# Routing of a two-stage mixture kernel: products of three token tiles taken together, gate steps of three chunks put behind the places

## What is computed

```python
# attention: B, H, S, D = 2, 8, 576, 64, causal softmax, plus a memory read, mixed by a gate
x = attn_out.transpose(0, 2, 1, 3).reshape(1152, 512)
h = x @ w_in                                   # 512 -> 2048
g = where(h >= 1, h, where(h <= -1, 0, (h + 1) ** 2 / 4))
x2 = g @ w_out                                 # 2048 -> 512
logits = x2 @ w_gate                           # 8 experts
expert_idx = argmax(logits, axis=1); gate_w = softmax(logits)[expert_idx]
for i in range(N):                             # a place in the expert's list, up to capacity 288
    e = expert_idx[i]
    if counts[e] < capacity: disp[e, counts[e]] = x2[i]; pos[i] = counts[e]; counts[e] += 1; keep[i] = True
y = relu(disp @ w1) @ w2
out[i] = gate_w[i] * y[expert_idx[i], pos[i]]  if keep[i] else 0
```

## Time and profile before

| | |
|---|---|
| median of 3 runs | 320.57 us (320.23 to 320.6) |
| profiled execution | 319.95 us, of it the traced span 318.2 us |
| TensorE matmul busy | 309.4 us (97% of the span), 2737 matmuls |
| VectorE busy | 212.0 us (67%) |
| ScalarE busy | 143.4 us (45%) |
| GpSimd busy | 122.3 us (38%) |
| granted TensorE clock | 1.00 (mean of the core), which is 2.4 GHz |

### The profile page before, as it was taken

One profiled execution on the slowest core, in us unless ns is written; L12 is line 12 of the kernel. 1 busy time (PEld: TensorE's weight loads), 2 busy tenths in 40 slices (PEclk: granted clock), 3 DMA queues, 4 the chain that ended last, 5 costly groups with the idle time before them and its releaser, 6 DMA issues.

```text
span 318.2 us, 7037 instructions
## 1 busy us (share of the span) xinstructions
PE 309.4 (97%) x2737; PEld 251.5 (79%) x2737; DVE 212.0 (67%) x569; ACT 143.4 (45%) x318; POOL 122.3 (38%) x146
## 2 busy tenths in 40 slices
PE   7999999999999999999999999999999999999994
PEld 6566676676677988878999989898989867775773
DVE  4899998999975576987856378567945465622300
ACT  1777875865965234555623343344434321101020
POOL 4777997998998100826850030003000000100031
PEclk9999999999999999999999999999999999999999
DMA  8999979951357400000003149420042075089820
GB/s 156 178 198 196 220 178 154 205 171 40 131 167 179 138 0 2 2 0 2 0 2 58 18 140 383 82 39 3 0 74 39 1 301 229 10 313 405 337 79 8
DMA packets 75047, 38.48 MB, mean 121 GB/s; under 512 B 66008, under 2 KB 66016, under 8 KB 73988
## 3 DMA queue, kind: packets, MB, share of 16 engines
q1 hardware_dynamic: 72340, 36.74, 43.9%
q10 hardware_dynamic: 2416, 0.59, 1.0%
q0 software_dynamic: 256, 0.67, 0.7%
HBM read 32.66 MB, written 5.39 MB: 120 GB/s over the span
## 4 chain that ended last, share of the span: by engine, by line
PE 92%; DVE 5%; issue 1%; POOL 1%; POOLq 0%; DVEq 0%
PE bank_a L1714 17%; PE bank_b L1714 13%; PE bank_out L1671 6%; PE bank_a L1572 4%; PE bank_b L1774 4%; PE bank_pt L1624 4%; PE bank_pt L1774 4%; PE bank_a L1648 3%; PE bank_b L1924 3%; PE bank_a L1924 3%; PE bank_b L1933 3%; PE bank_a L1933 3%; PE bank_b L1567 2%; PE bank_out L1747 2%; PE bank_out L1668 2%; PE bank_out L2061 2%
## 5 line engine op out<-in xcount | busy, mean ns | idle before, releaser
L683 POOL TENSOR_SCALAR prob<-prob,rl,gate_loc 128x512 f32<-128x512 f32 (+3 forms) x64 | 41.4, 662 | 12.0 <-DVE rl L1140 12.0
L1714 PE MATMUL bank_a<-x_hi,win_hi 128*128 128x288 f32 x128 | 39.3, 307 | 0.0
L1714 PE MATMUL bank_b<-x_hi,win_hi 128*128 128x288 f32 x128 | 38.1, 297 | 0.0
L1714 PE MATMUL bank_b<-x_lo,win_hi 128*128 128x288 f32 x128 | 38.0, 297 | 0.0
L1714 PE MATMUL bank_b<-x_hi,win_lo 128*128 128x288 f32 x128 | 38.0, 297 | 0.0
L1714 PE MATMUL bank_a<-x_hi,win_lo 128*128 128x288 f32 x128 | 38.0, 297 | 0.0
L1714 PE MATMUL bank_a<-x_lo,win_hi 128*128 128x288 f32 x128 | 38.0, 297 | 0.0
L712 POOL TENSOR_TENSOR x_lo<-xT,x_hi 128x1152 fp32r<-128x1152 f32 x4 | 10.6, 2660 | 64.7 <-ACT x_hi L869 64.7
L856 ACT ACTIVATE prob<-prob,negmax 128x512 f32<-128x512 f32 (+3 forms) x64 | 35.0, 548 | 0.8 <-DVE negmax L1090 0.8
L919 ACT ACTIVATE g_raw<-bank_a,biases 128x576 f32<-128x576 f32 x16 | 11.9, 742 | 51.2 <-DVE sq L1217 51.2
L1223 DVE TENSOR_TENSOR g_raw<-g_raw,sq 128x576 f32<-128x576 f32 x32 | 31.4, 981 | 0.9 <-ACT sq L920 0.5
(11 more groups left out here) (311 smaller groups left out, 757.3 us busy)
## 6 DMA issues: line engine op xcount, KB each, us to landing
w_sb<-in_moe_w_dram SPq DMA_DIRECT2D x6, 2048.0 KB, 13.5
win_raw<-in_moe_w_in_dram SPq DMA_DIRECT2D x4, 1024.0 KB, 5.9
wout<-in_moe_w_out_dram SPq DMA_DIRECT2D x4, 1024.0 KB, 5.7
win_raw<-in_moe_w_in_dram SPq DMA_DIRECT2D x1, 4096.0 KB, 13.7
out_dram<-zero_row SPq DMA_DIRECT2D x8, 288.0 KB
x_d<-x_rows SPq DMA_DIRECT2D x32, 72.0 KB, 2.1
v_sb<-in_v_dram SPq DMA_DIRECT2D x16, 128.0 KB, 2.6
qn<-in_q_dram SPq DMA_DIRECT2D x24, 72.0 KB, 5.6
```

The costliest lines, as they stand in the source:

```text
L683: pool.tensor_scalar(prob[u][:, h, :], prob[u][:, h, :], rl[:, c:c + 1], gate_loc[:, 2 * j + h:2 * j + h + 1], ALU.mult, ALU.mult).then_in ...
L1714: last = pe.matmul(h_bank(d)[:, t, :], w[:, m, f:f + P], x[c % 2][:, m, :], start=(m == 0 and n == 0), stop=(m == KT - 1 and n == 2))
```

## The change

`positions` now lays all three tiles out side by side in one group of 32 PSUM columns: three tiles of 8 and a fourth block that receives the totals. `ones` times `seen`, with `seen` repeated four times by an operand with a step of zero, covers all 32 columns. `before` times the `chosen` of all three tiles covers 24. Then `ones` times the `chosen` of tile r, repeated, covers the columns of all the later tiles and the totals: 24, 16 and 8 columns. Nine products become five. `ranks` is formed alike, nine products of one column become four of 3, 3, 2 and 1 columns, and the tenth product, that of the totals, is gone, since `positions` has them. The PSUM columns of the logits and of the first row's expert move to make room.

On VectorE the gate steps leave `place` and become `gates_of`. In routings 1 to 3 it runs at d = 7, that is behind `clip(c, 7)` and ahead of `add_terms(c, 6)`. In routing 4 it stays ahead of the places. In routing 1 the two steps `mtmp` and `mid` go behind `slot`. The step tables are rewritten to fit.

```diff
 
         CHOOSE = ("lg", "max", "eq", "pick", "idx", "chosen", "sub")
         GATE = ("sum", "eps", "gate", "tok", "exp", "p0", "rest0", "p1", "rest1", "p2")
-        LAST = ("lsum", "slotf", "slot", "slot_l", "lseen")
-        FIRST = CHOOSE + ("first_f", "first") + GATE + ("mgate", "prod", "pos", "csum", "seen", "hot", "hprod", "handled", "left", "over",
-                                                        "mtmp", "mid") + LAST + ("base", "listed")
-        NEXT = CHOOSE + GATE + ("prod", "pos", "csum", "seen", "bprod", "bsum", "pos2", "left", "over") + LAST + ("tot", "listed")
+        PLACE = ("left", "over", "lsum", "slotf", "slot")
+        END = ("slot_l", "lseen")
+        FIRST = CHOOSE + ("first_f", "first", "prod", "pos", "csum", "seen", "hot", "hprod", "handled") + PLACE + ("mtmp", "mid"
+                          ) + GATE + ("mgate",) + END + ("base", "listed")
+        MIDDLE = ("prod", "pos", "csum", "seen", "bprod", "bsum", "pos2") + PLACE
+        STEPS = (FIRST, CHOOSE + MIDDLE + GATE + END + ("tot", "listed"), CHOOSE + MIDDLE + GATE + END + ("tot", "listed"),
+                 CHOOSE + GATE + MIDDLE + END + ("tot", "listed"))
 
         def step_no(c, name):
 
-            return (FIRST.index(name) if c == 1 else len(FIRST) + (c - 2) * len(NEXT) + NEXT.index(name)) + 1
+            return sum(len(names) for names in STEPS[:c - 1]) + STEPS[c - 1].index(name) + 1
...
-            def place(c):
+            def gates_of(c):
 
                 dve.wait_ge(s_ex, c)
                 step(c, "sum", dve.tensor_reduce(total, ex[:, :, :], AX.X, ALU.add))
@@ -1332,6 +1336,9 @@
...
                 if c == 1:
                     step(c, "mgate", dve.tensor_copy(main_gate[:, :], of_row(c, 0)))
+
+            def place(c):
+
...
                     after(c, "handled")
                     step(c, "left", dve.tensor_scalar(left[:, :], handled, -1.0, 1.0, ALU.mult, ALU.add))
                     step(c, "over", dve.tensor_scalar(over, handled, float(NOWHERE), None, ALU.mult))
-                    step(c, "mtmp", dve.tensor_scalar(taken, handled, -float(NOWHERE), float(NOWHERE), ALU.mult, ALU.add))
-                    after(c, "mtmp")
-                    step(c, "mid", dve.tensor_tensor(main_id[:, :], taken, tok_f[:, 0:NR], ALU.add))
...
+                if c == 1:
+                    step(c, "mtmp", dve.tensor_scalar(taken, handled, -float(NOWHERE), float(NOWHERE), ALU.mult, ALU.add))
+                    after(c, "mtmp")
+                    step(c, "mid", dve.tensor_tensor(main_id[:, :], taken, tok_f[:, 0:NR], ALU.add))
...
@@ -1401,6 +1409,8 @@
                         choose(c)
                     if c > 0 and d == 6:
                         place(c)
+                    if c > 0 and d == 7:
...
                     if c > 0 and d == ND:
                         rank_tokens(c)
...
             copy_lt(NCH)
             choose(NCH)
+            gates_of(NCH)
             place(NCH)
...
+                pe.matmul(bank_o[0:ST, 0:(NR + 1) * E], ones[:, :], seen[:, :].unsqueeze(1).to_broadcast([ST, NR + 1, E]),
+                          start=True, stop=False)
+                pe.matmul(bank_o[0:ST, 0:NR * E], before[:, :], chosen[:, :, :].rearrange("p r e -> p (r e)"), start=False, stop=False)
                 for r in range(NR):
-                    parts = [(before, chosen[:, r, :]), (ones, seen[:, :])] + [(ones, chosen[:, o, :]) for o in range(r)]
-                    for n, (w, x) in enumerate(parts):
-                        last = pe.matmul(bank_o[0:ST, r * E:r * E + E], w[:, :], x,
-                                         start=(n == 0), stop=(n == len(parts) - 1))
+                    last = pe.matmul(bank_o[0:ST, (r + 1) * E:(NR + 1) * E], ones[:, :],
+                                     chosen[:, r:r + 1, :].to_broadcast([ST, NR - r, E]), start=False, stop=(r == NR - 1))
                 if c == 1:
-                    last = pe.matmul(bank_o[0:ST, 2 * NR * E:2 * NR * E + E], first_row[:, :], chosen[:, 0, :], start=True, stop=True)
+                    last = pe.matmul(bank_o[0:ST, HOT_AT:HOT_AT + E], first_row[:, :], chosen[:, 0, :], start=True, stop=True)
                 last.then_inc(s_pos, 1)
 
             def ranks(c):
 
                 pe.wait_ge(s_r, step_no(c, "over"))
-                for r in range(NR):
-                    parts = [(before, left[:, r:r + 1]), (ones, lseen[:, :])] + [(ones, left[:, o:o + 1]) for o in range(r)]
-                    for n, (w, x) in enumerate(parts):
-                        pe.matmul(bank_o[0:ST, 80 + r:81 + r], w[:, :], x, start=(n == 0), stop=(n == len(parts) - 1))
-                pe.matmul(bank_o[0:ST, 96:96 + E], ones[:, :], seen[:, :], start=True, stop=True).then_inc(s_rank, 1)
+                pe.matmul(bank_o[0:ST, 80:80 + NR], ones[:, :], lseen[:, 0:1].to_broadcast([ST, NR]), start=True, stop=False)
+                last = pe.matmul(bank_o[0:ST, 80:80 + NR], before[:, :], left[:, :], start=False, stop=False)
+                for r in range(NR - 1):
+                    last = pe.matmul(bank_o[0:ST, 81 + r:80 + NR], ones[:, :], left[:, r:r + 1].to_broadcast([ST, NR - 1 - r]),
+                                     start=False, stop=(r == NR - 2))
+                last.then_inc(s_rank, 1)
```

More of the change, by code:

```diff
@@ L622, in build_program @@
         list_ps = bank_o[:, 112:112 + PARTS]
+        LG_AT, HOT_AT = (NR + 1) * E, (2 * NR + 1) * E
         def s_bank(u):
@@ L1287, in choose @@
                 dve.wait_ge(s_lg, c)
-                step(c, "lg", dve.tensor_copy(lg[:, :, :], bank_o[0:ST, NR * E:2 * NR * E].rearrange("p (r e) -> p r e", e=E)))
+                step(c, "lg", dve.tensor_copy(lg[:, :, :], bank_o[0:ST, LG_AT:LG_AT + NR * E].rearrange("p (r e) -> p r e", e=E)))
                 after(c, "lg")
@@ L1343, in place @@
                 if c == 1:
-                    step(c, "hot", dve.tensor_copy(first_hot[:, :], bank_o[0:ST, 2 * NR * E:2 * NR * E + E]))
+                    step(c, "hot", dve.tensor_copy(first_hot[:, :], bank_o[0:ST, HOT_AT:HOT_AT + E]))
                     after(c, "hot")
@@ L1378, in rank_tokens @@
                 if c == 1:
-                    step(c, "base", dve.tensor_tensor(base[:, :], bank_o[0:ST, 96:96 + E], first_hot[:, :], ALU.mult))
+                    step(c, "base", dve.tensor_tensor(base[:, :], bank_o[0:ST, NR * E:NR * E + E], first_hot[:, :], ALU.mult))
                 else:
-                    step(c, "tot", dve.tensor_copy(tot, bank_o[0:1, 96:96 + E]))
+                    step(c, "tot", dve.tensor_copy(tot, bank_o[0:1, NR * E:NR * E + E]))
                 if c == 1:
@@ L1403, in chunk @@
                         place(c)
+                    if c > 0 and d == 7:
+                        gates_of(c)
                     if c > 0 and d == ND:
@@ L1787, in first_logits @@
                     for m in range(KT):
-                        last = pe.matmul(bank_o[0:ST, (NR + r) * E:(NR + r + 1) * E], x2T[:, m, r * ST:(r + 1) * ST], wg[:, m, :],
+                        last = pe.matmul(bank_o[0:ST, LG_AT + r * E:LG_AT + (r + 1) * E], x2T[:, m, r * ST:(r + 1) * ST], wg[:, m, :],
                                          start=(m == 0), stop=(m == KT - 1))
@@ L1798, in token_logits @@
                 for r in range(NR):
-                    last = pe.matmul(bank_o[0:ST, (NR + r) * E:(NR + r + 1) * E], lgT[:, r * ST:(r + 1) * ST], sel[:, 0:E],
+                    last = pe.matmul(bank_o[0:ST, LG_AT + r * E:LG_AT + (r + 1) * E], lgT[:, r * ST:(r + 1) * ST], sel[:, 0:E],
                                      start=True, stop=True)
```

## The result

The changed kernel took 316.64 us in the median of 4 runs (316.42 to 316.72), the kernel before 320.4 us beside it (4 runs, 320.2 to 320.6). The ratio is 0.9882, with a 95% interval of 0.9865 to 0.9899, so 3.8 us won where 3.2 were forecast.

The account below looks back on a forecast made before the run. TensorE was taken to bound the kernel: 1.80 us from 40 fewer products plus 1.47 from ended waits made 3.27, taken as 3.2, so 320.57 - 3.2 = 317.4 us. The range was 316.5 to 318.8.

Parts of the forecast that it names:

- What bounds the kernel: Whole kernel: TensorE, busy 97% of the span; only less TensorE work or ended TensorE waits, three at `ranks`, win time.
- The products that go: Positions and ranks: 10 products fewer in each of four routings, 40 at 45 ns, 1.80 us won on TensorE.
- The columns that come: Positions: 64 more moving columns per routing, taken to cost nothing, at most 0.25 us in four routings.
- A step of zero: Positions and ranks: operands repeated on TensorE, taken to cost nothing; 0.90 us if all 36 products left cost 70 ns.
- The rival of dear operands: Positions and ranks: products with a repeated operand cost 70 ns, not 45; gain 2.4 us, time 318.2; chance 0.10.
- the slower one: Positions and ranks: each product finishes before the next starts, 186 ns each; 1.8 us slower, 322.4; chance 0.03.
- The waits that go: Ranks of routings 1 to 3: TensorE's waits for `over` vanish completely, 0.61 and twice 0.43, 1.47 us won.
- Where the gate steps go: VectorE behind `clip(c, 7)`: 1.48 us of steps fit without a new wait; slack in routing 3 falls from 1.2 to 0.5.
- The tail: Kernel's end: last expert weights land by 303.3, needed about 311.6; their issue moves forward too, so nothing is given back.
- The sum: Whole kernel: 1.80 + 1.47 = 3.27 us won, taken as 3.2; 320.57 - 3.2 = 317.4 us.

Follow-up runs that it names:

- Both parts alone: Two runs against the kernel before (319.2 us): only the gate steps moved, 317.42 us, ratio 0.9943; only the small products changed, 317.38 us, ratio 0.9941.
- The products alone: The changed kernel with the gate steps back ahead of the places: 317.38 us against 319.2 for the kernel before, ratio 0.9941.
- the plain and the repeated products: The changed kernel plus ten unread products per position group, moving operand of 24 plain columns or 8 repeated: 318.48 and 318.45 us, ratios to before 0.9942 and 0.9944.
- Gate steps alone: The kernel before with the gate steps moved as in the change and its own products: 317.42 us against 319.2, ratio 0.9943.
- The longer gate steps: The changed kernel plus ten dependent VectorE steps behind the moved gate steps, routings 1 to 3: 318.77 us against 320.24 for the kernel before, ratio 0.9948.
- The second traces of the two kernels: Changed kernel rerun unaltered, 316.89 us against 320.24, ratio 0.9888; kernel before traced again on another occasion, 320.24 us.
- the wider matrices: The changed kernel with `ones` and `before` 128 columns wide: 314.54 us against 319.2 for the kernel before, ratio 0.9858; on another occasion 316.1 against 320.54, 0.9867.

## Why the prediction was right

- **What bounds the kernel** held: TensorE's work and its three waits set the time. Both parts alone gave what they take from TensorE's queue.
- **The products that go**, 1.80 us: right. From the first small product to the next big matmul, each of the four position groups is 0.18 us shorter, together 0.72. At the ranks, routing 4, where there never was a wait, gives 0.27 for six products (0.27 forecast). The products alone gave 1.8 to 1.9 us.
- **The columns that come**, nothing, with 0.25 us as bound: right, shown by the plain and the repeated products.
- **A step of zero**, nothing, with 0.90 us as bound: right. The rival of dear operands (318.2) and the slower one (322.4), in which each product waits for the last, are both ruled out by 45 ns.
- **The waits that go**, 1.47 us: the mechanism was right, the size too small. This is the step that missed. I took 0.22 us for the start of a small product behind a big one when nothing is waited for, from the `logits` in the earlier trace rows. It is 0.13. With that the waits are 0.70, 0.52 and 0.52, in all 1.74, and the second product follows after 0.03 and not 0.07, which is 0.1 more in three routings. Gate steps alone measured 1.8. The sum with these sizes is 1.80 + 1.74 + 0.1 = 3.64, and the place-by-place sum is 3.63. The `logits` were the wrong model. Why they start 0.09 us later was not tried. For the second product the trace of before had the right one, the ranks of routing 4, which wait for nothing: there it follows the first at once (270.39 behind 270.36), as it now does in all routings.

```profile
269.15 1.38 PE L1924 MATMUL bank_a<-x2T,w_sb 128*128 128x288 f32 x5
...
270.39 0.18 PE L1823 MATMUL bank_out<-lseen,ones 96*96 96x1 bf16 x1
```

For the first product routing 4 would have misled too. It stands 0.24 us behind the last of these five big matmuls, and that is also their distance from one another. The big matmuls of `hidden`, of line 1714, stand 0.13 apart (193.99 and 194.12 in the trace of before), and that is the distance at which the first product of the ranks now follows them. So in both places a small product that waits for nothing comes when the next big one would have come, and the number was to be had from the big matmuls' own distance. The `logits` behind them don't keep to this.

- **Where the gate steps go**: right, with 0.59 us of slack measured in place of 0.5. The longer gate steps showed that this slack is real and what takes over when it is used up. What I had called easier, the banks' release, is in truth the next limit of routing 1. I looked at the bank of `clip(c, 7)` and not at those of the next chunk, whose clips stand behind the moved steps. In routing 1 the room between ScalarE's end with `bank_a` and TensorE's next use of it fell from 2.4 us (199.95 + 0.74 to 203.10) to 1.4 (199.36 + 0.74 to 201.53), the last two lines being those of the changed kernel:

```profile
199.95 0.74 ACT L919 ACTIVATE g_raw<-bank_a,biases 128x576 f32<-128x576 f32 x1 [1.49 <-DVE sq L1217]
203.10 0.40 PE L1714 MATMUL bank_a<-x_hi,win_hi 128*128 128x288 f32 x1
...
199.36 0.74 ACT L923 ACTIVATE g_raw<-bank_a,biases 128x576 f32<-128x576 f32 x1 [2.87 <-DVE sq L1221]
201.53 0.40 PE L1725 MATMUL bank_a<-x_hi,win_hi 128*128 128x288 f32 x1
```

- **The tail** gave nothing back that belongs to the change. The second traces of the two kernels, though of two occasions, both have the pause. Their spans are 318.4 and 315.1, 3.3 us apart, and the lead behind the ranks of routing 4 is 3.1 (270.03 - 266.94).
- **The sum** was 3.27 and should have been 3.64. That is 0.37 of the 0.76 us by which 317.4 is too high; 0.07 more were rounded off, and 0.17 are the level of the kernel before (320.4 in place of 320.57). The medians differ by 3.8 us the first time and by 3.35 the second (320.24 - 316.89), to both sides of the 3.63 of the traces and within the intervals. The working also gave 316.75 for an execution like the profiled one, and the profiled one took 316.72. That is luck: 0.37 us of lead from before the routings and 0.37 missing in the sum are made up for by the pause of 0.8.

On the price of a small product the runs decide between page and page. The Trainium skill, TensorE: Matmul & The Clock Gate, section LDWEIGHTS, prices a load by its columns, which would have the wider matrices dearer, 128 / 1.2 = 107 ns against 80, an estimate from that page. The trace disagrees for products in a row: 25 ns against 45. The section Weight-path perf modes of that page of the Trainium skill says that fast weight load is on when the number of weights is 128 and the type is not fp32. The trace agrees with that as far as the two distances go, 25 ns with 128 columns and 45 with 96.

## What to carry over

When one engine is the bound, count its small instructions: each costs its distance to the next, here 45 ns with 1 to 24 moving columns, and a repeated operand lets one product do the work of several. Before moving work behind a wait, read what the other engine's queue has behind the new place, with its slack in us, since that slack is what the move may use and is testable by putting in dummy steps. Take the cost of a hand-over without a wait from a place where nothing waits and where the same two instructions meet. Where there is none, the distance of the big instructions from one another (here 0.13 us) was a better guess than another pair (0.22 or 0.24).

## What had not been expected of the hardware

A bf16 product with 96 stationary columns costs 45 ns in a row of them, one with 128 costs 25 to 26. Padding the small stationary matrices to 128 columns took 0.5 us out of the kernel by its traces.

A small product that waits for nothing starts behind a big matmul at the big ones' own distance, 0.13 us behind those of `hidden` and 0.24 behind those of the first expert.

80 semaphore increments on TensorE's queue took 12.1 us, 0.15 us each, over three times a small product.
